# Row maxima of attention scores: one reduce over both halves of a tile

## The reference

```
scores = scale * q @ k.T                     # 4 x 8 heads of 576 x 64
thresh = max(scores, -1) - tau
scores = where(scores >= thresh, scores, -1e9)
attn   = softmax(scores)
x      = (attn @ v) arranged as 2304 x 512
x      = ((x @ w_a) * (x @ w_b)) @ w_out      # 512 -> 1536 -> 512
h      = x @ w_in                             # 512 -> 1024
out    = layernorm(h * softmax(h)) * g @ w_out2
```

## Time and profile before

| | |
|---|---|
| median of the timed runs | 1056.58 us |
| span of the profiled execution | 1053.5 us |
| what lies around the span (the difference of the two) | 3.1 us |
| PE busy | 1000.4 us, 95% |
| DVE busy | 609.5 us, 58% |
| ACT busy | 446.5 us, 42% |
| POOL busy | 271.7 us, 26% |
| the 320 reduces of L711 | 130.9 us of DVE, 449 ns each |
| PE in the chain that ended last | 81% of the span |
| DVE in that chain | 11% |

### The profile page before, as it was taken

The page is one execution under the profiler, slowest core; times in us unless marked ns, Lnnn a source line. Parts: engine busy times, 40 slices in busy tenths (PEclk is TensorE's granted clock), DMA queues, the critical chain, the costliest instruction groups (busy, mean ns, idle before and its releaser), DMA issues.

```text
span 1053.5 us, 17281 instructions
## 1 busy us (share of the span) xinstructions
PE 1000.4 (95%) x5936; PEld 931.2 (88%) x5936; DVE 609.5 (58%) x1125; ACT 446.5 (42%) x771; POOL 271.7 (26%) x220
## 2 busy tenths in 40 slices
PE   5998998999899899999999999999999999999998
PEld 5887887888888789999999999999999978888886
DVE  7899999999999975421121221221213576666564
ACT  5777777777777754421121211211213423222231
POOL 3776776677677640000000000000000000000000
PEclk9999999999999999999999999999999999999999
DMA  6655655655565335200000000000001200000000
GB/s 156 150 138 138 153 138 145 153 140 137 141 153 130 102 103 172 90 1 2 1 0 0 0 0 0 0 0 0 0 2 78 80 11 31 20 20 20 20 30 30
DMA packets 43259, 70.67 MB, mean 67 GB/s; under 512 B 10398, under 2 KB 14622, under 8 KB 43228
## 3 DMA queue, kind: packets, MB, share of 16 engines
q1 hardware_dynamic: 43228, 70.28, 25.4%
HBM read 33.10 MB, written 4.79 MB: 36 GB/s over the span
## 4 chain that ended last, share of the span: by engine, by line
PE 81%; DVE 11%; issue 5%; ACT 1%; DMA 1%; DVEq 0%; SPq 0%; POOL 0%; POOLq 0%; ACTq 0%
PE PS L1012 9%; PE PS L1014 9%; PE PS L1013 9%; PE PS L995 8%; PE PS L1073 5%; PE PS L1072 5%; PE PS L1071 5%; DVE neg_max L711 3%; PE PS L965 3%; PE PS L1130 3%; PE PS L1132 3%; PE PS L1131 3%; PE PS L951 3%; PE PS L952 3%; PE PS L1106 3%
## 5 line engine op out<-in xcount | busy, mean ns | idle before, releaser
L435 POOL TENSOR_TENSOR p_lo<-prob,p_hi 128x576 fp32r<-128x576 f32 x128 | 182.5, 1436 | 100.3 <-ACT p_hi L495 98.7
L1012 PE MATMUL PS<-x_hi,w_ab_rolled 128*128 128x384 f32 x576 | 192.6, 334 | 1.3 <-DVE w_ab_rolled L755 1.3
L1014 PE MATMUL PS<-x_hi,w_ab_rolled 128*128 128x384 f32 x576 | 192.4, 334 | 0.0
L1013 PE MATMUL PS<-x_lo,w_ab_rolled 128*128 128x384 f32 x576 | 192.4, 334 | 0.0
L818 DVE TENSOR_TENSOR gate<-gate,PS 128x384 f32<-128x384 f32 x72 | 39.9, 554 | 258.1 <-ACT gate L596 258.1
L596 ACT ACTIVATE gate<-PS 128x384 f32<-128x384 f32 x72 | 35.4, 491 | 264.9 <-PE PS L1014 264.9
L711 DVE TENSOR_REDUCE neg_max<-PS 128x1 f32<-128x288 f32 (+1 forms) x320 | 130.9, 449 | 25.2 <-PE PS L952 22.0
L729 DVE SCALAR_TENSOR_TENSOR prob<-PS,neg_tau,prob 128x576 f32<-128x576 f32 (+1 forms) x160 | 126.4, 806 | 1.1 <-ACT prob L487 1.1
L487 ACT ACTIVATE prob<-PS 128x576 f32<-128x576 f32 (+1 forms) x160 | 103.6, 647 | 40.6 <-PE PS L966 40.2
L455 POOL MEMSET halfpow<- 128x1 f32 x1 | 0.1, 98 | 447.6 <-PE PS L1073 447.6
L495 ACT ACTIVATE p_hi<-prob 128x576 fp32r<-128x576 f32 (+1 forms) x160 | 105.9, 680 | 14.0 <-DVE prob L729 11.2
(11 more groups left out here) (92 smaller groups left out, 1875.5 us busy)
## 6 DMA issues: line engine op xcount, KB each, us to landing
qk_raw<-qkT_dram SPq DMA_DIRECT2D x32, 288.0 KB, 3.0
ops<-qk_hi SPq DMA_DIRECT2D x62, 144.0 KB
ops<-qk_hi SPq DMA_DIRECT2D x31, 288.0 KB
ops<-qk_lo SPq DMA_DIRECT2D x62, 144.0 KB
v_raw<-v_tiles_dram SPq DMA_DIRECT2D x32, 160.0 KB, 2.2
xT<-head_sb SPq DMA_DIRECT2D x32, 144.0 KB, 2.4
inverse_all<-inverse_dram SPq DMA_DIRECT2D x32, 144.0 KB, 3.1
out_dram<-o_sb SPq DMA_DIRECT2D x18, 256.0 KB, 2.0
```

The costliest lines, as they stand in the source:

```text
L435: pool.tensor_tensor(dst, prob[0:n, r, :], p_hi[0:n, r, :].bitcast(F32), ALU.subtract).then_inc(p_lo_done, 1)
L1012: pe.matmul(bank, w[:, 0, :], x_hi[:, k, :], start=(k == 0), stop=False)
L1013: pe.matmul(bank, w[:, 0, :], x_lo[:, k, :], start=False, stop=False)
L1014: ins = pe.matmul(bank, w[:, 1, :], x_hi[:, k, :], start=False, stop=(k == NK - 1))
```

## The change

Each tile gets one reduce over both halves (`axis` XY, input 2 x 288) in place of one for each half, and writes straight to `neg_max`. `neg_max2` is gone, and so are both minima. A `tensor_copy` of `neg_max` makes the high part in `max_cols`. `scores` now signals once for a tile, after its fourth matmul, and waits once for a tile, ahead of its first, for the reduce of the tile before.

```diff
-            dve.memset(neg_max2[:, :, :], 0.0).then_inc(ones_set, 1)
+            dve.memset(neg_max[:, :], 0.0).then_inc(ones_set, 1)
...
-                for b in range(2):
-                    dve.wait_ge(s_done, 2 * (NT * h + t) + b + 1)
-                    dve.tensor_reduce(out=neg_max2[0:n, b, t:t + 1], in_=ps[0:n, b, 0:HALF],
-                                      axis=AX_X, op=ALU.max, negate=True).then_inc(max_done, 1)
+                dve.wait_ge(s_done, NT * h + t + 1)
+                dve.tensor_reduce(out=neg_max[0:n, t:t + 1], in_=ps[0:n, :, 0:HALF],
+                                  axis=AX_XY, op=ALU.max, negate=True).then_inc(max_done, 1)
...
-                dve.wait_ge(max_done, 2 * NT * (h + 1))
+                dve.wait_ge(max_done, NT * (h + 1))
                 at_least(dve, max_turned, h)
-                dve.tensor_tensor(neg_max[:, :], neg_max2[:, 0, :], neg_max2[:, 1, :], ALU.min)
-                dve.tensor_tensor(max_cols[:, :, 0], neg_max2[:, 0, :], neg_max2[:, 1, :], ALU.min).then_inc(max_hi_done, 1)
+                dve.tensor_copy(max_cols[:, :, 0], neg_max[:, :]).then_inc(max_hi_done, 1)
                 dve.wait_ge(max_hi_done, h + 1)
...
-                    at_least(pe, max_done, 2 * (t - 2))
+                    at_least(pe, max_done, t - 2)
...
+                if t > 0 and ps is s_ps:
+                    at_least(pe, max_done, NT * h + t)
                 for b in range(2):
-                    if t > 0 and ps is s_ps:
-                        at_least(pe, max_done, 2 * (NT * h + t - 1) + b + 1)
                     cols = slice(b * HALF, (b + 1) * HALF)
                     pe.matmul(ps[0:n, b, 0:HALF], qq[:, r, tile_cols(t)], kk[:, r, cols], start=True, stop=False)
-                    pe.matmul(ps[0:n, b, 0:HALF], qx[:, r, tile_cols(t)], kx[:, r, cols],
-                              start=False, stop=True).then_inc(s_done, 1)
+                    ins = pe.matmul(ps[0:n, b, 0:HALF], qx[:, r, tile_cols(t)], kx[:, r, cols],
+                                    start=False, stop=True)
+                ins.then_inc(s_done, 1)
```

More of the change, by code:

```diff
@@ L21 @@
 AX_X = mybir.AxisListType.X
+AX_XY = mybir.AxisListType.XY
 P = 128
@@ L103, in build_program @@
             inverse_all = sb(a, "inverse_all", [P, 2, S])
-            neg_max2 = sb(a, "neg_max2", [P, 2, NT])
             neg_max = sb(a, "neg_max", [P, NT])
```

## The result

The changed kernel took 1070.4 us (median of 4 runs, 1069.7 to 1070.8) against 1056.4 for the kernel before: 14.0 us or 1.32% slower (ratio 1.0132, 95% interval 1.012 to 1.0144). The forecast was 1065.7, with a range of 1058.5 to 1070.5.

A forecast was written before the change was run, and what follows sets the result against it. No engine is full in the attention part; a loop through DVE, PE and POOL bounds each step. Terms 7.7, 2.5, 0.5, -0.9, -0.6 and -0.1 sum to +9.1 us: 1065.7 us, range 1058.5 to 1070.5.

The forecast's parts named there:

- The reduce: On DVE, one reduce of 576 elements takes 0.75 us where two halves take 0.82, 0.07 less per tile.
- The wait for both halves: Maxima wait for a tile's fourth matmul: +0.50 us in each of 18 steps without normalize, -0.07 in 13 with it.
- The copy held by POOL: In the split, POOL's second subtraction holds the copy; split ends at P + 3.03: +0.20, 0 or -0.08 us a step.
- rival A: In the split, the copy is not held and splits end at P + 2.83: +2.9 us, 1059.5 us; chance 0.17.
- D: More lost: reduce at 0.82 (2.5 and 0.9 us), then p_hi(2) delaying POOL's second subtraction (1.5); 1070.5 us, upper end of 0.68.
- Steps with normalize: 13 steps: -0.07 us each from the reduce, and -0.08 in 8 of them from the split.
- The start: Head 0's five maxima: gains of 0.07 us each and a later fourth tile about cancel, -0.1 us.
- B: DVE's count decides: each tile saves 0.07 us and each split 0.08, 13.7 us faster, 1042.9 us; chance 0.06.
- C: The split slips between POOL's two subtractions; each step loses about 1.2 us of waiting, about 1028 us; chance 0.03.

The follow-up runs named there:

- coarse_waits: Kernel before with scores signalling and waiting once for a tile; still two reduces, both minima and no copy: 1079.4 us.
- early_scores: Changed kernel with the next head's first tile of scores moved ahead of the last two matmuls of values in PE's queue: 1068.6 us.
- free_copy: Changed kernel with the copy alone made by tensor_reduce; the subtract with two SBUF inputs stays: 1065.1 us.
- head0_bank: Changed kernel with the fourth tile of head 0 in the bank of the values, so PE doesn't wait for the third maximum: 1069.4 us.
- free_split: Changed kernel with copy and subtract both made by tensor_reduce, three instructions with one SBUF input each: 1035.8 us.
- half_free: Kernel before, its two reduces and half-wise waits kept, with the split made by four tensor_reduce instructions: 1022.2 us.

## Why the prediction was right, and where it was short

The sign and the mechanism held, and the time fell inside the range, 0.1 us from its end. The size was 9.1 us where 14.0 were measured. By its own steps:

- *The reduce*: forecast 0.75 us, measured 0.752.
- *The wait for both halves*: forecast +0.50 at mask(0) in steps without normalize, measured +0.55. In those with normalize forecast -0.07, measured -0.07. coarse_waits shows the wait alone to be the cause, early_scores that its chain passes on what is put into it.
- *The copy held by POOL*: forecast held, split end at P + 3.03. Held in 31 of 31 steps (mean 1.30 us, the free one of head 0 included). free_copy priced rival A's case at 5.3 us, where the two sums of the forecast differ by 6.2. In steps without normalize P to split end was 3.10 and not 3.03, since POOL's second subtraction often starts late: the pair lasts 2.92 us at 48.00, for one, where it lasted 2.80. In the mean it is 0.06 longer in these steps and 0.04 in those with normalize, 1.5 us in all. That was the second term of D, and its price.
- *Steps with normalize*: forecast -1.5 us in all, measured -1.0. The 0.08 where L718 had been the long one was mostly used up by POOL's longer pair; P to split end is 3.08 before and after.
- *The start*: the step that failed. Forecast -0.1 for the maxima of head 0 and +0.4 for the first step, measured +1.5 and +2.0. The forecast let a later fourth tile and five gains of 0.07 cancel. The fourth tile starts 0.80 later, over twice the gains, and head0_bank, which takes that wait away, has its first split where the kernel before has it. It also took the pace of PE as given, and in this execution the lower level lasted 11 us longer. Why it did is open. The pause isn't shown to be the reason.

The sum put together again: start 1.5, first step 2.0, 17 steps 12.5, 13 steps -1.0, behind the last split -0.5, in all 14.5 us of span. Against the forecast that is 3.2 us more at the start, 2.2 in the 17 steps and 0.5 in the 13, and 0.5 less behind the last split.

*The rivals.* B (DVE's count decides) fell: DVE did 14.3 us less and the kernel took 14.0 more. Fewer instructions paid only where DVE is behind PE, in the steps with normalize (0.07 us each). C didn't occur by itself. Its estimate that a split free of POOL is worth some 1.2 us a step was near: free_split and half_free show 34.6 and 34.3 us for 31 steps. D's value is where the time came out, but not by its terms. Of its 4.9 us the 3.4 for a reduce of 0.82 us did not come (it took 0.752), the 1.5 for POOL's second subtraction did, and the start, which D does not name, made up most of the rest. That the time still lies in the range is luck.

## What to carry to other kernels

Two small instructions that each follow their half of a producer's work are worth more than one long one, if the consumer waits for the producer and the producer for the consumer: look for idle time ahead of the instruction before merging, and price the later start at both ends of the handshake. A tiny instruction with a mean many times its usual length is waiting for something. Here that was POOL, in every step, and taking the split out of POOL's way was worth more than twice the loss that was being explained.

## What was not expected of the hardware

- A 128x5 copy with a stride of 128 elements in its output is held by POOL as fully as an instruction with two inputs: 1.39 us against 0.16 for the same copy made by tensor_reduce at the same place.
- At the start TensorE's level went up and down more than once (in head0_bank up at 11.2 us, down at 14.6, up at 18.0; in half_free up at 10.1, down at 17.0, up at 20.4), with a granted clock of 0.50 in between. Two kernels with the same instructions and the same pause up to 10.8 us had it up at 10.4 us and at 21.3. What decides it stays open.
- A granted clock of 1.00 at the start of a trace can mean that there is no record yet. The spacing of the matmuls, 0.24 or 0.13 us, told the two levels apart.
